# Attention through 32 inducing points and two MLPs on one core: batch `h @ w_in` in four partition quarters, its parts cut in three steps and put into rows by DMA, with the first MLP's first units beside the second batch's join

## The reference

```python
B, N, C = x.shape            # 2, 12480, 128
m = inducing.shape[0]        # 32
def mab(q, kv):
    s = scale * (q @ kv.transpose(0, 2, 1))
    s = s - s.max(-1, keepdims=True)
    a = np.exp(s)
    a /= a.sum(-1, keepdims=True) + 1e-09
    return a @ kv
h = mab(I, x)                # 32 rows per batch
attn = mab(x, h)             # every token against its batch's 32 rows
# first MLP: w_in 128x2048, w_out 2048x128
h = x @ w_in
P = a[0] + a[1] * h + a[2] * h2 + a[3] * h3
Q = 1.0 + np.abs(b[0]) * np.abs(h) + np.abs(b[1]) * h2
g = P / (Q + 1e-06)
y = g @ w_out
# second MLP, its own weights: (h * cos(h)) @ w_out, h = y @ w_in
```

## Time and profile before

| | us |
|---|---|
| median of 3 runs | 2629.5 (2629.24 to 2630.69) |
| the profiled execution | 2632.91 |
| its span | 2631.1 |
| PE busy in the span | 2584.3 (98%) |
| ACT, DVE, POOL busy | 2423.3, 2341.6, 2052.3 |
| mean granted clock of PE | 0.989 |

### The profile page before, as it was taken

How to read it: one execution, slowest core, us unless ns; L and a number is a source line. 1 busy time by engine, 2 the same in 40 slices (tenths; PEclk the granted TensorE clock), 3 DMA queues, 4 the chain that set the end, 5 groups by cost and what they waited for, 6 DMA issues and landing times.

```text
span 2631.1 us, 38615 instructions
## 1 busy us (share of the span) xinstructions
PE 2584.3 (98%) x10691; PEld 1794.6 (68%) x10691; DVE 2341.6 (89%) x2730; ACT 2423.3 (92%) x3173; POOL 2052.3 (78%) x1474
## 2 busy tenths in 40 slices
PE   8699999999999999999999999999999999999999
PEld 5366656665666666665656688888888888888887
DVE  4599999999999999999999888888888888888887
ACT  5499999999999999999999899999999999999998
POOL 0189999999999999999999777777777777777776
PEclk9699999999999999999999999999999999999999
DMA  7000000000002000000000000000000000000000
GB/s 220 21 8 11 10 8 11 7 11 7 11 17 71 8 11 7 11 8 11 7 11 5 1 12 12 12 11 11 11 11 11 11 11 11 11 11 11 11 11 15
DMA packets 25688, 45.52 MB, mean 17 GB/s; under 512 B 2888, under 2 KB 11880, under 8 KB 25384
## 3 DMA queue, kind: packets, MB, share of 16 engines
q1 hardware_dynamic: 25640, 44.92, 5.7%
HBM read 16.99 MB, written 12.78 MB: 11 GB/s over the span
## 4 chain that ended last, share of the span: by engine, by line
PE 62%; POOL 14%; issue 10%; DVE 8%; ACT 4%; DMA 1%; POOLq 1%; DVEq 0%; ACTq 0%; SPq 0%
PE bank L1166 22%; PE bank L1158 20%; POOL work L379 8%; PE bank L1016 8%; PE bank L1023 8%; DVE work L776 5%; POOL work L367 3%; POOL part_hi L389 2%; ACT work L532 2%; DVE bank L758 1%; PE bank L947 1%; PE bank L1149 1%; ACT work L520 1%; POOL part_hi L383 1%; DVE work L767 1%
## 5 line engine op out<-in xcount | busy, mean ns | idle before, releaser
L446 POOL TENSOR_TENSOR act_lo<-work,act_hi 128x960 fp32r<-128x960 f32 (+1 forms) x416 | 723.4, 1744 | 330.1 <-ACT act_hi L607 322.1
L1023 PE MATMUL bank<-work,v 128*128 128x480 f32 x1664 | 742.5, 568 | 0.2 <-ACT tokens_t L539 0.2
L1016 PE MATMUL bank<-part_hi,stack_now 96*128 96x480 f32 x2496 | 665.0, 400 | 13.7 <-DVE stack_next L704 7.1
L379 POOL TENSOR_TENSOR work<-work 128x960 f32<-128x960 f32 x278 | 621.9, 2237 | 42.3 <-POOL work L367 3.4
L912 DVE SCALAR_TENSOR_TENSOR work<-work,bank 128x960 f32<-128x960 int32 x416 | 479.6, 1153 | 155.3 <-ACT work L594 155.3
L1016 PEld LDWEIGHTS bank<-part_hi,stack_now 96*128 96x128 f32 x2496 | 434.9, 189 | 241.8 <-DVE work L776 161.9
L758 DVE SCALAR_TENSOR_TENSOR bank<-bank,over_c,work 128x960 f32<-128x960 f32 x416 | 508.4, 1222 | 42.8 <-PE bank L1016 34.1
L776 DVE SCALAR_TENSOR_TENSOR work<-bank,coef_a,work 128x960 f32<-128x960 f32 x416 | 502.2, 1207 | 0.2 <-PE bank L1016 0.2
L515 ACT ACTIVATE work<-work,made 128x960 f32<-128x960 f32 x416 | 469.1, 1128 | 26.2 <-POOL work L379 26.2
L594 ACT ACTIVATE work<-bank 128x960 int32<-128x960 f32 x416 | 404.2, 972 | 93.1 <-PE bank L1158 93.1
L918 DVE TENSOR_TENSOR work<-work,bank 128x960 f32<-128x960 f32 x416 | 477.2, 1147 | 0.0
(11 more groups left out here) (120 smaller groups left out, 3039.3 us busy)
## 6 DMA issues: line engine op xcount, KB each, us to landing
x_group<-tokens_t SPq DMA_DIRECT2D x52, 240.0 KB, 2.2
out_dram<-work SPq DMA_DIRECT2D x52, 240.0 KB, 2.4
x_ring<-in_x_dram SPq DMA_DIRECT2D x40, 240.0 KB, 6.1
work<-in_x_dram SPq DMA_DIRECT2D x12, 240.0 KB, 4.0
stack_now<-stack_next SPq DMA_DIRECT2D x8, 288.0 KB, 3.0
work<-in_moe_w_in_dram SPq DMA_DIRECT2D x1, 1024.0 KB, 15.4
w_raw<-in_moe_w_in_dram SPq DMA_DIRECT2D x1, 1024.0 KB, 4.9
v<-in_moe_w_out_dram SPq DMA_DIRECT2D x2, 0.5 KB, 13.9
```

Of the source, the lines that this page charges most:

```text
L379: nc.gpsimd.tensor_tensor(quot[k % 3], square[k % 3], abs_h[k % 3], ALU.add).then_inc(den_ready, 1)
L446: nc.gpsimd.tensor_tensor(act2_lo[:, k % 2, w], angle[k % ANGLES][:, w], act2_hi[:, k % 2, w].bitcast(F32), ALU.subtract).then_inc(act2_pa ...
L1016: mm = pe.matmul(place_out[:, t, :], stack_now[:, i, w], part_hi[0:K3, place, :], start=start, stop=stop, skip_group_check=not start)
L1023: mm = pe.matmul(sums, v[:, 2 * u + t, :], g[:, t * GROUP:(t + 1) * GROUP], start=(2 * u + t == 0), stop=(2 * u + t == CHUNKS - 1))
```

## The change

- `fold` multiplies `ht` (32 columns, kept once now) by a quarter of `w_in` into one partition quarter of one bank, four quarters in two calls. Thus the product lies as 128 partitions x 512 instead of 96 x 2048.
- ACT rounds it by three instructions, one for each coefficient, and DVE takes the low part by three, into `first_hi` and `first_lo`, or `next_hi` and `next_lo` for batch 1.
- SP puts them into `stack_now`'s three sets of 32 rows: for batch 0 12 DMAs (8 of high parts, 4 of low) in stage one, for batch 1 three for each unit's columns at the change of batch, where one was.
- The second group's softmax moves into stage one's loop, and so do the first two `hidden`; the next units' work is interleaved with batch 1's join.
- `w_raw` has a place of its own, `x_ring` 8 slots instead of 12 (the other 8 in `work`), the sums of `sum_h` go to bank 5, and batch 1's join to bank 6. Waits follow suit.

The diff, cut to its core:

```diff
-RING_NEXT = 12
+RING_NEXT = 8
...
-        stack_next = sb("stack_next", [K3, 3, F], F32R)
+        next_hi = sb("next_hi", [P, 3, PIECE], F32R)
+        next_lo = sb("next_lo", [P, 3, PIECE], F32R)
...
-        w_raw = work[:, 10 * UNIT - F:]
+        w_raw = at(rest_at, "w_raw", [P, F])[:, :]
+        first_hi = at(work_at, "first_hi", [P, 3, PIECE], F32R)
+        first_lo = at(work_at + 12 * UNIT, "first_lo", [P, 3, PIECE], F32R)
+        parts_hi, parts_lo = [first_hi, next_hi], [first_lo, next_lo]
...
-        join = [bank[:, 7, :], bank[:, 5, :]]
-        pieces = [[3, 5, 3, 5], [2, 3, 4, 5]]
+        join = [bank[:, 7, :], bank[:, 6, :]]
+        folded = [bank[:, 3, :], bank[:, 7, :]]
...
+            def first_stack(rows, part):
+                for j in range(PIECES):
+                    sp.dma_start(stack_now[rows * M:(rows + 1) * M, :, j * PIECE:(j + 1) * PIECE].bitcast(F32),
+                                 part[j * M:(j + 1) * M, :, :].bitcast(F32)).then_inc(stack_first, 16)
...
             def next_stack(u):
-                sp.dma_start(stack_now[:, :, w].bitcast(F32), stack_next[:, :, w].bitcast(F32)).then_inc(stack_ready[u], 16)
+                for rows, part in ((0, next_hi), (1, next_lo), (2, next_hi)):
+                    sp.dma_start(stack_now[rows * M:(rows + 1) * M, :, w].bitcast(F32),
+                                 part[j * M:(j + 1) * M, :, c:c + 2 * P].bitcast(F32)).then_inc(stack_ready[u], 16)
...
             fetch_group(1)
+            sp.wait_ge(stack_hi, STACKS)
+            first_stack(0, first_hi)
+            first_stack(2, first_hi)
+            sp.wait_ge(stack_lo, STACKS)
+            first_stack(1, first_lo)
...
+            def fold_hi(batch, i):
+                act_.wait_ge(folded_in, batch + 1)
+                nc.scalar.activation(parts_hi[batch][:, i, :], folded[batch], ACT.Identity, scale=fold_scale[i]).then_inc(stack_hi, 1)
...
                 if k == BATCH_STEPS + 9:
                     s2_exponent(0)
+                    act_.wait_ge(scales_step, 7)
+                    fold_hi(0, 0)
+                    fold_hi(0, 1)
+                if k == BATCH_STEPS + 10:
+                    fold_hi(0, 2)
...
+            def fold_lo(batch, i):
+                dve.wait_ge(stack_hi, (batch + 1) * STACKS)
+                nc.vector.scalar_tensor_tensor(out=parts_lo[batch][:, i, :], in0=folded[batch], scalar=fold_scale[i],
+                                               in1=parts_hi[batch][:, i, :].bitcast(F32), op0=ALU.mult, op1=ALU.subtract).then_inc(stack_lo, 1)
...
+                if k == BATCH_STEPS + 11:
+                    fold_lo(0, 0)
+                    fold_lo(0, 1)
+                if k == BATCH_STEPS + 12:
+                    fold_lo(0, 2)
...
-            def fold(batch, piece):
+            def fold(batch, js):
+                for j in js:
+                    mm = pe.matmul(folded[batch][j * M:(j + 1) * M, :], ht[:, batch, :], w_raw[:, j * PIECE:(j + 1) * PIECE], start=True, stop=True)
...
+                if k == STEPS:
+                    pe.wait_ge(xt_ready, GROUPS)
+                    pe.wait_ge(stack_first, 16 * PIECES * 3)
+                    hidden(0, 0)
...
+                    fold(0, range(PIECES // 2))
                     score2(0, 0, range(GROUP_SUBS))
...
+                if k == BATCH_STEPS + 8:
+                    fold(0, range(PIECES // 2, PIECES))
```

More of the change, by code:

```diff
@@ L287, in bass_set_attention_two_mlps, with later @@
         block = ctx.enter_context(nc.Block())
-        folds = [(batch, i, 2 * pair + h) for batch in range(B) for pair in range(PIECES // 2) for i in range(3) for h in range(2)]
-        BATCH_FOLDS = len(folds) // B
         fold_scale = [made[:, 1:2], over_c2[:, 1:2], coef_a[:, 1:2]]
+        STACKS = len(fold_scale)
+        def later(group):
+            return exists(group) and not (isinstance(group, int) and group < 2)
         @block.sync
@@ L497, in weigh_stream @@
                                      scale=SCALE).then_inc(weight_ready, 1)
-            def fold_hi(step):
-                batch, i, piece = folds[step]
-                act_.wait_ge(folded_in, batch * PIECES + piece + 1)
-                if step >= 2:
-                    act_.wait_ge(stack_lo, step - 1)
-                stack = (stack_now, stack_next)[batch]
-                nc.scalar.activation(stack[:, i, piece * PIECE:(piece + 1) * PIECE], bank[0:K3, pieces[batch][piece], :], ACT.Identity,
-                                     scale=fold_scale[i][0:K3]).then_inc(stack_hi, 1)
+            def fold_hi(batch, i):
+                act_.wait_ge(folded_in, batch + 1)
+                nc.scalar.activation(parts_hi[batch][:, i, :], folded[batch], ACT.Identity, scale=fold_scale[i]).then_inc(stack_hi, 1)
             def s2_exponent(g):
@@ L851, in _ @@
                     step_bias(k - 1)
-            unit(0, MAX[0] + GROUP_UNITS)
+                if k == STEPS:
+                    max_s2(1, 1)
+                    shift_s2(1, 1)
+                if k == STEPS + 2:
+                    sum_s2(1, 1)
+                    invert(1, 1)
             weigh_sum(1)
-            units(0, range(-MAG - 1, -MAG + 1))
+            absolute(0, 1)
+            product(0, 0)
             choose(1)
-            unit(0, -MAG + 1)
+            keep_att(1, 1)
             keep_ht(1)
-            for step in range(BATCH_FOLDS, 2 * BATCH_FOLDS):
-                fold_lo(step)
-            units(0, range(-MAG + 2, 1))
+            absolute(0, 2)
+            unit(0, -1)
+            for i in range(STACKS):
+                fold_lo(1, i)
+            unit(0, 0)
             with dve.Fori(0, W2_LOOP) as i:
@@ L1031, in score2 @@
                 for j in subs:
-                    mm = pe.matmul(spare[0:SUB, j * M:(j + 1) * M], x_group[:, j * SUB:(j + 1) * SUB], ht3[:, batch, 0, :], start=True, stop=True)
+                    mm = pe.matmul(spare[0:SUB, j * M:(j + 1) * M], x_group[:, j * SUB:(j + 1) * SUB], ht[:, batch, :], start=True, stop=True)
                 if subs[-1] == GROUP_SUBS - 1:
```

126 lines of the change are left out of this document (63 added, 63 removed).

## The result

The changed kernel takes 2620.39 us (median of 6 runs, 2619.84 to 2622.37), the kernel before on the same chip 2630.10 (6 runs, 2626.67 to 2633.42): ratio 0.9964, 95% interval [0.9952, 0.9977]. That is 9.7 us faster, with 6.0 to 12.6 for the interval. The forecast was 2613.5, with a range of 2608 to 2621.5. The profiled execution took 2620.76 us.

What follows compares the result with a forecast made beforehand. PE was taken as the bound, so only time won before the first MLP's loop counts: 5.9 us from part 1 plus 10.1 from part 3 make 16.0; 2632.9 - 16.0 - 3.4 = 2613.5 us, range 2608 to 2621.5.

Steps and rivals of the forecast that it cites:

- Step 21: Starting mark on PE in stage one, its first transpose at 71.94 us; nothing ahead of it was to be shortened.
- Part 1: Batch 0's fold and parts in stage one: 20.0 us from step 21 to the last scores, 5.9 us won.
- the last scores: Mark on PE at the end of stage one's scores: 97.93 us before, forecast at about 92.0.
- The wait for the twelve transfers: PE's wait in front of the first `hidden` for batch 0's stack rows moved by DMA: 1.5 us.
- The rival of slow 32-partition transfers: Few partitions move slowly: 1.42 us a transfer, a wait of 9.5 us, time 2621.5; chance 0.18.
- One by one: Rival: each of the 12 transfers lands before the next, PE waits 27.5 us, time 2639.5; chance 0.04.
- Part 3: Units beside batch 1's join, last scores to slope 3: 30.2 us with the DMA wait, 10.1 us won.
- slope 3: Slope of unit 3, the mark where both kernels start the same loop: 138.20 us before, forecast at 122.2.
- given back: Rival: units beside the join add their work uncovered, 7.9 us, time 2618, or 2626 with slow transfers; chance 0.06.
- Quarters overlap: Its rival: quarters don't overlap and half clock stays, a fold pair takes 3.7 us, time 2618.5; chance 0.12.
- Full clock behind slope 3: From slope 3 on both kernels were taken to run the same loop; the sum had no term for it.
- At the batch change: Three transfers replace each one, at most 1.2 us more to issue, with 16 us of room: no cost.

Runs made afterwards that it cites:

- The probe: A kernel that computes no part of the reference and only moves data within SBUF in groups of transfers, the changed kernel's twelve first; 135.54 us in one run.
- r8: Changed kernel with the first two `hidden` and DVE's first magnitude moved behind the spread of batch 1's peak; 2614.72 us, ratio 0.9944.
- r7: Changed kernel with four repeated products with `w_out` in PE's idle time in front of slope 3; 2621.33 us, ratio 0.9964.
- r1: The changed kernel again, unaltered, as a yardstick; 2622.62 us, ratio 0.997.
- r2: Changed kernel with the twelve transfers sorted by column quarter, a semaphore each, so the first `hidden` waits for three; 2618.6 us, ratio 0.9955.
- r6: Changed kernel with only the order of the twelve transfers altered, so that neighbours lie on different halves of the partitions; 2621.71 us, ratio 0.9966.
- r10: The same kernel as r8, run again as a yardstick; 2615.27 us, ratio 0.994.
- r9: Changed kernel with four more transfers of 128 KB between the high and low ones, the first `hidden` waiting for them too; 2623.52 us, ratio 0.9975.
- r3: Changed kernel with DVE's product of unit 2 and quotient of unit 1 ahead of batch 1's three low parts; 2621.86 us, ratio 0.997.
- r4: Changed kernel with the edits of r2 and r3 together; 2617.86 us, ratio 0.9955.
- r12: r8 with r3's order on DVE and four repeated matmuls in PE's idle stretches of the join; 2613.97 us, ratio 0.9935.

## Why the prediction was right or wrong

The sign was right and the range held the time, but the point was 6.9 us too low. By the prediction's own sign of being wrong, a wait of more than 5 us for the twelve transfers, it failed: PE waits 5.72. That the time stayed in the range is in part luck, as the sum at the end shows. Step by step:

- **Step 21** was to stand at 71.94 and stands at 70.87. In the twelve traces it stands anywhere from 69.3 to 73.4, so this 1.1 us can't be put down to the change.
- **Part 1** was right: 20.0 us from step 21 to the last scores in the sum, 90.59 - 70.87 = 19.7 in the trace, and 19.3 to 20.7 in all twelve. Quarters run side by side (1.03 and 1.06 us for a pair at full clock), and a part of 512 columns on 128 partitions costs what a piece of 512 on 96 or 32 did: 0.68 to 0.69 us on ACT, 0.74 to 0.75 on DVE. The last scores came at 90.59, and at 91.3 as a mean of the twelve traces, for a forecast of 92.0.
- **The wait for the twelve transfers was the step that failed**: 1.5 us forecast, 5.72 measured. I took 0.71 us a transfer by scaling the old copy's bytes; the stretches of the changed kernel have 0.90. Twelve then move for 10.8 us and not 8.5. From the first issue (82.92) to `hidden(0)` (97.29) it takes 14.4 us for 10.0 in the sum, so 2.3 of the missing 4.4 are moving. The other 2.1 lie beside it: no byte moves before 84.0, `hidden` starts some 1.2 us behind the last ones (about 96.1), and what moves between amounts to 2.63 MB, where the twelve are 2.36. Nearly all the rest is group 2's `x_group` fetch (0.25 MB), issued at 93.19 and called harmless in the sum. The probe's twelve, with no fetch behind them, took 13.3 us from the first issue to SP's next, so up to 1.1 us of the wait may be the fetch's; no run takes it away, so this is not shown. (The first issue came 1.6 us sooner than forecast and the last scores 1.4, which nearly cancels.)
- **The rival of slow 32-partition transfers** was thus the true mechanism at a smaller size: it had 9.5 us by the nearest rows (10.0 with the 0.5 to report that the sum itself has). By the Trainium skill, "SBUF — State Buffer", section "Door 1: The DMA port swizzle", partitions 0 to 31 reach half of the ports and gave 189 GB/s; that estimate had a wait of 5.0 and 2617.0 (5.5 and 2617.5 with the 0.5 to report), nearer than my sum. The traces agree in kind, with 207 to 215 GB/s for its 189. On 128 partitions they show 299, held back by issue, for its 328. I had given that rival 0.18; with the page's numbers beside a trace that had no such transfer, it deserved most of the chance.
- **One by one** is refuted: all twelve take 14.4 us, though one takes 4.6 us to land in the median, so several are under way at once.
- **Part 3** without the wait was 30.2 - 1.5 = 28.7 us from last scores to slope 3, and took 33.0 - 5.7 = 27.3. The way to the spread's end cost 9.4 without the wait (9.3 forecast), from there to the first fold of `ht` 6.6 (7.4), from that fold to slope 3 11.4 (12.0). The gain is not given back by the units: r8 prices them at 2.8 us at most against the 3.8 that they save. Quarters overlap at half clock too (1.92 for a pair), so that rival falls as well.
- **Full clock behind slope 3 was assumed, and was wrong.** PE idles 3.82 us in front of it, and the clock falls to half from about 123 to 129 us. From slope 3 to the last product it takes 1349.6 us for 1347.0: 2.6 us that the sum did not have. r7, which fills the idle time, gets 2.0 of them back. I had looked at what is late next, and not at what the idle PE does to its clock.
- **At the batch change** nothing is lost: no wait of PE for the stack, and the loop still at 3.25 us a unit.

Sum in the traces: 16.0 forecast, less 4.2 (wait), less 2.6 (clock), plus 1.4 (part 3) and 1.4 (last scores, 1.1 of them ahead of step 21) is 12.0, the measured difference of the last products. The last two terms offset errors that have nothing to do with them, which is luck: without their 2.8 us the same two errors would have put the time near 2623, outside the range. The remaining 3.0 us of the error lie in the last step, "2632.9 - 16.0 - 3.4". I took off the 3.4 us by which the profiled execution of before stood over its median as if both kernels had them; the changed kernel's profiled execution stands 0.4 over its own. So the traced difference of 12 overstates what the medians show, 9.7, and where the profiled execution of before lost its microseconds stays open, as no second trace of it was taken.

## What to carry to other kernels

Before work is moved onto DMAs, price them by the partitions that they touch, not by bytes alone: 32 partitions at a time moved at 207 to 220 GB/s here, 128 at 299. Let work that does not need them stand ahead of the wait: with the same transfers, two units moved behind batch 1's last steps won 5 us or more (ratios to the kernel before of 0.9944 and 0.994 for 0.9964 and 0.997), since on an in-order engine a wait holds up whatever is queued behind it. And when a stall in front of a loop is shortened or moved, look at the stretch behind it too, since the granted clock may charge for the idle time.

## What the runs showed of the hardware

- The share of the 16 DMA engines reads as saturated (1.04 to 1.09) at 214 as at 261 GB/s. A share near one is no rate.
- How long PE idled in front of slope 3 and what the clock did: after 3.7 to 3.8 us it fell in the changed kernel, r1, r2 and r6; after 2.88 us it fell in r10, and after 1.65 us it stayed up in r8, which is the same kernel; after 1.57 us it stayed up in r9. So one kernel can meet both, and a single trace doesn't price a clock effect. With almost equal waits (0.99 and 1.40 against 1.07 and 1.40) it fell in r3 and not in r4, two kernels that differ in the transfers' order. Against 1347.0 to 1347.3 us of rest where it stayed up, the rest was 1348.1 in r10, 1349.6 in the changed kernel and 1353.9 in r3 (its two waits included).
- In r8 PE is at half clock from 94 to 114 us, although from 98 to 114 its stretches add up to 14.7 busy us of 16. In r12, with its four repeats, it stays at full until 106 us, 14 us behind the last scores, where r8's is down 6 us behind them.
